# Down-projections of two steps at a time as seven block products (steps 16 to 27 and 40 to 47), and the finished parts of the up weights kept in DRAM for a second use

## What is computed

```python
a = a / (np.sum(a, axis=-1, keepdims=True) + 1e-09)
x = np.matmul(a, v_all)                       # 2 x 8 heads, 768 tokens -> 1536 x 512
...
for e in range(E):                            # E = 4, w1 512 x 1024, w2 1024 x 512
    h = np.maximum(x @ w1[e], 0.0)
    out += p[:, e:e + 1] * (h @ w2[e])
...
h = x @ w_in                                  # 512 x 2048
g = h * (1.0 / (1.0 + np.exp(-1.702 * h)))
return g @ w_out                              # 2048 x 512
```

## Time and profile before

| what | us |
|---|---|
| median of 3 runs | 838.62 (838.14 to 839.32) |
| the profiled execution, its own time | 837.34 |
| its span, first to last instruction | 835.6 |
| PE busy in the span | 814.5 (97%) |
| POOL, DVE, ACT busy | 556.5, 537.9, 399.3 |

### The profile page before, as it was taken

One profiled execution on the slowest core, in us unless ns is written; L12 is line 12 of the kernel. 1 busy time (PEld: TensorE's weight loads), 2 busy tenths in 40 slices (PEclk: granted clock), 3 DMA queues, 4 the chain that ended last, 5 costly groups with the idle time before them and its releaser, 6 DMA issues.

```text
span 835.6 us, 13851 instructions
## 1 busy us (share of the span) xinstructions
PE 814.5 (97%) x5014; PEld 800.9 (96%) x5014; DVE 537.9 (64%) x1194; ACT 399.3 (48%) x859; POOL 556.5 (67%) x414
## 2 busy tenths in 40 slices
PE   5889999999999999999999999999999999999998
PEld 4688999999999999999999999999999999999998
DVE  6888656666655665665665665665665666666665
ACT  3865454444454454433434344444555554554541
POOL 3688655656655799566566588787488787466450
PEclk9989999999999999999999999999999999999999
DMA  9945233142211122122122121121122122321102
GB/s 281 281 126 189 90 117 106 51 153 74 97 52 70 51 84 89 51 76 95 51 82 90 51 88 65 51 93 59 51 74 79 50 82 72 126 86 67 51 1 76
DMA packets 26420, 74.72 MB, mean 89 GB/s; under 512 B 14704, under 2 KB 15856, under 8 KB 20208
## 3 DMA queue, kind: packets, MB, share of 16 engines
q1 hardware_dynamic: 26352, 73.84, 26.9%
HBM read 70.66 MB, written 3.17 MB: 88 GB/s over the span
## 4 chain that ended last, share of the span: by engine, by line
PE 90%; POOL 3%; ACT 3%; issue 2%; DVE 2%; DMA 1%; SPq 0%; DVEq 0%; ACTq 0%; POOLq 0%
PE bank L1155 29%; PE bank L1157 29%; PE bank L1156 29%; ACT prob L676 1%; PE bank L1110 1%; PE bank L1147 1%; PE bank L1121 1%; DMA v_cols<-v_t 1%; POOL wu_lo L536 1%; POOL wd_lo L548 1%; DVE masked L889 0%; POOL xb_other_lo L572 0%; DVE v_sum L877 0%; POOL wd_lo L564 0%; ACT xb_first_hi L737 0%
## 5 line engine op out<-in xcount | busy, mean ns | idle before, releaser
L957 DVE TENSOR_TENSOR xa<-bank,xa 128x384 f32<-128x384 f32 x352 | 195.8, 557 | 219.9 <-PE bank L1157 215.5
L1155 PE MATMUL bank<-h_hi,wd_hi 128*128 128x384 f32 x768 | 257.3, 335 | 0.3 <-DVE xa L955 0.2
L1157 PE MATMUL bank<-h_lo,wd_hi 128*128 128x384 f32 x768 | 256.7, 334 | 0.0
L1156 PE MATMUL bank<-h_hi,wd_lo 128*128 128x384 f32 x768 | 256.6, 334 | 0.0
L548 POOL TENSOR_TENSOR wd_lo<-stage,wd_hi 128x1024 fp32r<-128x1024 f32 x47 | 113.1, 2406 | 165.5 <-ACT wd_hi L719 165.5
L760 ACT ACTIVATE h_hi<-bank 128x384 fp32r<-128x384 f32 x192 | 94.5, 492 | 230.6 <-DVE bank L990 183.3
L1155 PEld LDWEIGHTS bank<-h_hi,wd_hi 128*128 128x128 f32 x768 | 144.2, 188 | 2.4 <-issue 1.5
L1156 PEld LDWEIGHTS bank<-h_hi,wd_lo 128*128 128x128 f32 x768 | 144.2, 188 | 0.0
L1157 PEld LDWEIGHTS bank<-h_lo,wd_hi 128*128 128x128 f32 x768 | 144.2, 188 | 0.0
L536 POOL TENSOR_TENSOR wu_lo<-stage,wu_hi 128x1024 fp32r<-128x1024 f32 x47 | 113.9, 2424 | 0.2 <-ACT wu_hi L707 0.2
L1155 PE MATMUL bank<-xb_other_hi,wu_hi 128*128 128x384 f32 x336 | 112.3, 334 | 0.3 <-ACT snap L744 0.3
(11 more groups left out here) (79 smaller groups left out, 1271.3 us busy)
## 6 DMA issues: line engine op xcount, KB each, us to landing
stage<-weights SPq DMA_DIRECT2D x48, 1024.0 KB, 4.9
k_win<-k_w SPq DMA_DIRECT2D x8, 720.0 KB, 7.7
v_win<-v_w SPq DMA_DIRECT2D x8, 576.0 KB, 8.7
q_bd<-q_t SPq DMA_DIRECT2D x16, 192.0 KB, 8.2
p_bc<-p_rows SPq DMA_DIRECT2D x8, 384.0 KB, 4.8
v_cols<-v_t SPq DMA_DIRECT2D x6, 384.0 KB, 5.9
out<-xa SPq DMA_DIRECT2D x4, 384.0 KB, 7.6
out<-xa SPq DMA_DIRECT2D x8, 192.0 KB, 1.9
```

The costliest lines, as they stand in the source:

```text
L957: nc.vector.tensor_tensor(at, y_bank(g, t), at, ALU.add).then_inc(y_taken, 1)
L1155: nc.tensor.matmul(dst, w_h, a_h, start=first, stop=False, skip_group_check=True)
L1156: nc.tensor.matmul(dst, w_l, a_h, start=False, stop=False, skip_group_check=True)
L1157: return nc.tensor.matmul(dst, w_h, a_l, start=False, stop=last, skip_group_check=True)
```

## The change

In steps 16 to 27 and 40 to 47 two consecutive steps (an even and the odd one after it) make a pair. Their hidden features together are a 512 x 512 factor, so that the down-projection of both can be done as seven block products too, each in two halves of output features d = 0, 1: 14 blocks of six matmuls (`pair_product`) in place of 16 (`down`). In the odd step of a pair PE does P1 and P5 of the pair between its up products, in the even step after it P3, P6, P2, P7 and P4. Around it:

- `gate` writes the tile to SBUF (`h_raw`) and no longer in place in its bank. ACT makes high parts of the raw tiles (`high_tile`, 6 per pair) and DVE the low ones (`low_tile`), POOL makes four sums of hidden blocks (`sum_hidden`, 128 x 768), ACT and DVE split these (`high_sum`, `low_sum`).
- POOL makes four sums of down-weight blocks per pair (`sum_held`, 128 x 512, in `stage`), ACT and POOL split seven held blocks (`high_held`, `low_held`), in place of `high_down` and `low_down`.
- A result block goes from its bank into `xa` 14 times a pair (`take_product`) and not 16.
- The high and low parts of the up weights of steps 1 to 15 and 32 to 39 are written to DRAM (`store_up`, two transfers of 917 KB a step), and read back for steps 17 to 31 and 40 to 47 (`load_up`), so that ACT and POOL make none there (`sum_weights`, `high_raw`, `low_raw`, `high_sums`, `low_sums` fall away). `load_weights` brings only the down half (512 KB) there.
- The blocks `xb_first` and `xb_last`, which hold the input blocks of phases 0 and 2, hold the hidden blocks of the pairs in phases 1 and 3. So those of phase 2 are prepared in three steps (29 to 31) and not six (26 to 31).
- The down weights of steps 29 and 30 are prepared both in step 29, those of 28 in step 28, 31 in 30.

```diff
-AHEAD = (None, 3, 6, 6)
+AHEAD = (None, 3, 3, 6)
...
+PAIRED = ((MOE_STEPS, 28), (FFN0 + PAIRS_2, STEPS))
...
+TAKES = (("P1", 0), ("P1", 1), ("P5", 0), ("P5", 1),
+         ("P3", 0), ("P3", 1), ("P6", 0), ("P6", 1), ("P2", 0), ("P7", 0), ("P7", 1), ("P2", 1), ("P4", 0), ("P4", 1))
+IN_PAIR = 4
...
+ADDED = {"P1": (0, 0, True), "P5": (1, 1, True), "P3": (0, 1, True), "P6": (0, 1, False), "P2": (0, 0, False),
+         "P7": (1, 1, False), "P4": (1, 0, True)}
+
+HELD_2 = ("P1", "P5", "P3", "P6", "P2", "P7", "P4")
+
+TILES_2 = ((0, "C11"), (0, "C21"), (1, "C11"), (1, "C22"), (1, "C21"), (1, "C12"))
...
+        def down_due(g):
+
+            due = [x for x in (g, g + 1) if x < STEPS and not paired(x)]
+            return [x for x in due if (x == g) == (x > 0 and (paired(x - 1) or (x > 1 and paired(x - 2))))]
...
             def load_weights(g):
 
-                wait_count(sp, dnlo_done, g - 1)
-                sp.dma_start(stage[:, g % 2, :], weights[weight_of(g), :, :]).then_inc(stage_in[g % 2], 16)
+                if g > 1:
+                    if paired(g - 2):
+                        sp.wait_ge(slo_done, len(HELD_2) * (pair_of(g - 2) + 1))
+                    else:
+                        sp.wait_ge(dnlo_done, plain(g - 2))
...
+            def load_up(g):
+
+                sp.wait_ge(up_done, ups(g - 2))
+                before = g - (MOE_STEPS if g < FFN0 else PAIRS_2)
+                sp.wait_ge(wu_stored[g % 2], 32 * max(stores(before), stores(g - 2)))
+                sp.dma_start(wu_hi[:, g % 2, :].bitcast(F32), split[weight_of(g), 0, :, :]).then_inc(wu_in[g % 2], 16)
+                sp.dma_start(wu_lo[:, g % 2, :].bitcast(F32), split[weight_of(g), 1, :, :]).then_inc(wu_in[g % 2], 16)
...
+            def sum_held(g):
+
+                n = 4 * pair_of(g)
+                a11, a12, a22, a21 = (held_source(p) for p in ("P1", "P2", "P4", "P5"))
+                for s in range(2):
+                    pool.wait_ge(stage_in[s], 16 * (g // 2 + 1))
+                nc.gpsimd.tensor_tensor(held_source("P7"), a11, a21, ALU.subtract).then_inc(ssum_done, 1)
+                pool.wait_ge(ssum_done, n + 1)
+                nc.gpsimd.tensor_tensor(a21, a21, a22, ALU.add).then_inc(ssum_done, 1)
+                pool.wait_ge(ssum_done, n + 2)
+                nc.gpsimd.tensor_tensor(held_source("P6"), a21, a11, ALU.subtract).then_inc(ssum_done, 1)
+                pool.wait_ge(ssum_done, n + 3)
+                nc.gpsimd.tensor_tensor(held_source("P3"), a12, held_source("P6"), ALU.subtract).then_inc(ssum_done, 1)
+
+            def low_held(g, name):
...
+            def sum_hidden(g, n):
+
+                at = 4 * pair_of(g)
+                if n == 1:
+                    pool.wait_ge(gated_done, ready(g, "C12"))
+                    wait_count(pool, tlo_done, at - 2)
+                    wait_count(pool, tsum_done, at)
+                    a, b = hidden_block(0, 1), hidden_block(0, 0)
+                elif n == 2:
+                    pool.wait_ge(gated_done, ready(g + 1, "C12"))
+                    pool.wait_ge(tlo_done, at + 1)
+                    a, b = hidden_block(1, 1), hidden_sum(1)
+                elif n == 3:
+                    pool.wait_ge(tsum_done, at + 1)
+                    a, b = hidden_block(1, 1), hidden_block(0, 1)
+                else:
+                    pool.wait_ge(tsum_done, at + 2)
+                    pool.wait_ge(blo_done, len(TILES_2) * pair_of(g) + TILES_2.index((1, "C21")) + 1)
+                    a, b = hidden_block(1, 0), hidden_sum(2)
+                nc.gpsimd.tensor_tensor(hidden_sum(n), a, b, ALU.subtract).then_inc(tsum_done, 1)
+
             spread_key_maxima(0)
...
+                if second(g):
+                    sum_hidden(g - 1, 1)
+                    low_held(g - 1, "P3")
+                    low_held(g - 1, "P6")
+                    low_held(g - 1, "P2")
+                    low_held(g - 1, "P7")
+                    low_held(g - 1, "P4")
+                elif paired(g - 1):
+                    sum_hidden(g - 2, 2)
+                    sum_hidden(g - 2, 3)
+                    sum_hidden(g - 2, 4)
...
+                if paired(g) and not second(g):
+                    sum_held(g)
+                    low_held(g, "P1")
+                    low_held(g, "P5")
...
+                for x in down_due(g):
+                    low_down(x)
...
+            def high_tile(g, c):
+
+                g0 = g - g % 2
+                act.wait_ge(gated_done, ready(g, c))
+                if paired(g0 - 1):
+                    act.wait_ge(y_done, taken(g0 - 2, {(0, "1"): "P1", (1, "1"): "P2", (1, "2"): "P3"}[g % 2, c[2]], 1))
+                else:
+                    act.wait_ge(up_done, ups(g0 - 1))
+                nc.scalar.activation(moved_tile(g, c)[0], hidden_raw(g, c), ACT.Copy).then_inc(bhi_done, 1)
...
+            def high_sum(g, n):
+
+                act.wait_ge(tsum_done, 4 * pair_of(g) + n)
+                if paired(g - 1):
+                    act.wait_ge(y_done, taken(g - 2, ("P5", "P6", "P7", "P4")[n - 1], 1))
+                else:
+                    act.wait_ge(up_done, ups(g - 1))
+                nc.scalar.activation(moved_2(n + 1)[0], hidden_sum(n), ACT.Copy).then_inc(thi_done, 1)
...
+            def low_tile(g, c):
+
+                dve.wait_ge(bhi_done, len(TILES_2) * pair_of(g) + TILES_2.index((g % 2, c)) + 1)
+                hi, lo = moved_tile(g, c)
+                nc.vector.tensor_tensor(lo, hidden_raw(g, c), hi.bitcast(F32), ALU.subtract).then_inc(blo_done, 1)
+
+            def low_sum(g, n):
+
+                dve.wait_ge(thi_done, 4 * pair_of(g) + n)
+                hi, lo = moved_2(n + 1)
+                nc.vector.tensor_tensor(lo, hidden_sum(n), hi.bitcast(F32), ALU.subtract).then_inc(tlo_done, 1)
...
+            def pair_product(g, name, d):
+
+                n = len(TILES_2) * pair_of(g)
+                if name in ("P1", "P2", "P3"):
+                    pe.wait_ge(blo_done, n + {"P1": 2, "P2": 5, "P3": 6}[name])
+                else:
+                    pe.wait_ge(tlo_done, 4 * pair_of(g) + {"P5": 1, "P6": 2, "P7": 3, "P4": 4}[name])
+                pe.wait_ge(slo_done, len(HELD_2) * pair_of(g) + HELD_2.index(name) + 1)
+                if name in ("P1", "P5"):
+                    pe.wait_ge(y_taken, taken(g - 2, {"P1": "P4", "P5": "P2"}[name], d) if paired(g - 1) else takes(g))
+                else:
+                    pe.wait_ge(y_taken, taken(g, {"P3": "P5", "P6": "P3", "P2": "P3", "P7": "P6", "P4": "P7"}[name], d))
+                hi, lo = moved_2(MOVED[name])
+                w_hi, w_lo = held_2(name)
+                for f in range(2):
+                    w = slice(BW * f + P * d, BW * f + P * (d + 1))
+                    last = three(pair_bank(name, d), w_hi[:, w], w_lo[:, w], hi[:, f, :], lo[:, f, :],
+                                 name in ("P1", "P5", "P2") and f == 0, f == 1)
                 last.then_inc(y_done, 1)
 
...
+                if second(g):
+                    product(g, "P1")
+                    pair_product(g - 1, "P1", 0)
+                    product(g, "P2")
+                    product(g, "P5")
+                    product(g, "P6")
+                    pair_product(g - 1, "P1", 1)
+                    product(g, "P7")
+                    pair_product(g - 1, "P5", 0)
+                    product(g, "P4")
+                    pair_product(g - 1, "P5", 1)
+                    product(g, "P3")
+                    continue
+                if paired(g - 1):
+                    product(g, "P1")
+                    product(g, "P2")
+                    product(g, "P5")
+                    pair_product(g - 2, "P3", 0)
+                    product(g, "P6")
+                    pair_product(g - 2, "P3", 1)
+                    pair_product(g - 2, "P6", 0)
+                    product(g, "P7")
+                    pair_product(g - 2, "P6", 1)
+                    pair_product(g - 2, "P2", 0)
+                    pair_product(g - 2, "P7", 0)
+                    product(g, "P4")
+                    pair_product(g - 2, "P7", 1)
+                    pair_product(g - 2, "P2", 1)
+                    pair_product(g - 2, "P4", 0)
+                    product(g, "P3")
+                    pair_product(g - 2, "P4", 1)
+                    continue
                 product(g, "P1")
                 down(g - 1, 0)
...
-            for t in range(8):
-                down(STEPS - 1, t)
+            for name, d in TAKES[IN_PAIR:]:
+                pair_product(STEPS - 2, name, d)
```

More of the change, by code:

```diff
@@ L860, in _ @@
                     act.wait_ge(table_in, 1)
+            for n in (2, 3, 4):
+                high_sum(STEPS - 2, n)
         @block.vector
@@ L1078, in _ @@
                 take_y(g - 1, 6)
-                low_hidden(g, "C22")
-                low_hidden(g, "C21")
+                if paired(g):
+                    low_tile(g, "C21")
+                else:
+                    low_hidden(g, "C22")
```

(1 more changed line is left out.)

410 lines of the change are left out of this document (340 added, 70 removed).

## The result

The changed kernel takes **846.36 us** in the median (844.79 to 848.16, four runs), the kernel before 838.53 us on the same chip (838.14 to 839.32): a ratio of 1.0101, 95% interval 1.0082 to 1.0119. The prediction was 847.0, range 834 to 856. The profiled execution took 844.79 us, with a span of 842.9 against 835.6.

The account below looks back on a forecast made before the run. PE's matmul count was taken as the bound: -20.8 us for removed matmuls, +7.5, +7.3, +6.0, +4.4, +1.6 and +3.0 for waits and clock, +9.0 in sum; 846.3 for the profiled execution, 847 forecast for the median, range 834 to 856.

Parts of the forecast that it names:

- The sum: Whole kernel: all gains and losses add to +9.0 us on the profiled 837.3, plus 1.3 for the median over that execution.
- What bounds the kernel: Middle of the kernel: only the number of matmuls on PE sets the time, six matmuls per 1.04 us block.
- Turns between DVE and POOL: DVE operations with two SBUF inputs and POOL instructions each wait for the other's whole instruction; ten meet 15 per pair.
- The steady pair: Even steps 18 to 28: PE waits 1.0 us at P3, 0.1 and 0.2 at P6 and P7; +7.5 us in all.
- being 0.4 late from turns in that step: Odd step of a pair: DVE reaches `add_c12` at 12.0 us, 0.4 late, so `gate` ends at 13.1.
- Steps 42 to 46: Steps 42, 44, 46: a sigmoid delays `gate`; PE waits 2.15 us at P3, 0.3 behind; 2.4 each, +7.3.
- The end, and step 30: After the last up product: P3 5.3 us late, P6 1.1, net +6.0; `down(29, 0)` waits for low down weights, +4.4.
- Steps 31 and 32: Step 31: `sum_weights` of step 32 starts 6.3 us in, ACT's `high_raw` delays `keep`, PE's P7 waits; +1.6 us.
- In step 30 POOL runs on late: Step 30: `low_down` until 23.4 us, then five operations of 1.85, make POOL late for the up weights of step 32.
- The clock: After the two long stops of 4.4 and 5.3 us, PE runs at half clock, 1.5 us lost each; +3.0.
- Transfers: Reloads of up parts: due 12.4 us after being asked for, landing in 9, covered by 3.4 us; cost nothing.
- The rival of late up weights: Nine even steps wait for reloads that exceed 12.4 us; at 14.4 that is +18, 865 us; chance 0.1.

## Why the prediction was right

**The sum.** 847 against 846.4, and in the profiled execution +9.0 against +7.3. The largest single errors are 3.1 us in steps 18 to 28 and 1.8 in steps 42 to 46, both too much, and the end has 0.9 too much; they are met by 3.2 us that it did not have (step 42's transfer, the start, the 0.1 behind each stop, less the stop gone in step 16), by 0.4 more of half clock and by the 0.6 that is missing in the table's sum. The 1.3 us that the prediction added for the median over the profiled execution came out too, as 1.6, and no term of it says why it should. So that the two medians agree within 0.6 us is luck; that the terms add up to within 1.7 us is not, for each long stop is where it was put.

**What bounds the kernel.** Right: PE at its pace. With no sums on POOL the six P3 stops of steps 18 to 28, 4.4 us, are gone and the profile is 4.4 us shorter there; with up products ahead other stops took their place, and the gain is what was left.

**Turns between DVE and POOL.** Right, and shown: with the sums on 8 columns, and with the sum put behind the low part, the low part of C12 takes 0.56 in place of 1.71 to 1.75. In the second POOL still makes its sums in full, only later, so it is not their work but their time that counts. The trace shows the end of DVE's operation 0.4 us behind the end of POOL's, and the rule of the Trainium skill ("SBUF — State Buffer", section "SBUF: two separate sides") that a DVE operation with two SBUF inputs and POOL exclude each other for the whole instruction agrees. It works both ways: POOL is held as well, 2.56 for 1.85.

**The steady pair.** The place was right (P3, all six steps), the size not: 0.70 in place of 1.0 and no wait at P6 and P7. The step that was off is "being 0.4 late from turns in that step": `gate` ends at 383.60, 12.9 into the odd step, not 13.1, and from there on POOL, ACT and DVE run as worked out. P6 and P7 had been given 0.1 and 0.2, which is less than the same error.

**Steps 42 to 46.** 2.15 was expected at P3; 1.17 is measured there, and 1.0 in 44 and 46 at up P5, which waits for the gate behind the sigmoid. I had followed the gate's lateness only to P3, past a product that waits for it sooner: a mis-sized term at P3 and a missing place, whose sum is 2.17. In step 42 it is the late reload that PE waits for in place of the gate.

**The end, and step 30.** 5.4 and 4.2 us against 5.3 and 4.4: both were worked out from the order of instructions and the rows of before, and both vanish with the edit that takes their cause. P6 was given 1.1 more at the end and doesn't wait.

**Steps 31 and 32.** The number was right (1.6 against 1.7), and so was the last part of the chain: POOL comes to `sum_weights` of step 32 at 563.47, 5.97 us into step 31 (6.3 was said), ACT waits for it in `high_raw`, and `keep`, which PE needs, stands behind that:

```profile
563.47 0.74 POOL L700 TENSOR_TENSOR w_sum<-stage 128x256 f32<-128x256 f32 x1
```

```profile
565.05 1.06 ACT L961 ACTIVATE wu_hi<-stage 128x1024 fp32r<-128x1024 f32 x1 [5.42 <-POOL stage L702]
566.02 0.47 ACT L1019 ACTIVATE h_hi<-bank 128x384 fp32r<-128x384 f32 x1
566.38 0.48 ACT L1003 ACTIVATE snap<-bank 128x384 f32<-128x384 f32 x1
```

What fell is why POOL is late, "In step 30 POOL runs on late", behind the late weights of step 29: the 5.97 stands in the kernel without pairs and in that with early down weights as well. In all of them POOL first waits 3.1 us for ACT's high part of a moved block, which stands behind the high parts of that step's tiles and down weights, and so keeps PE's pace; before, with the moved blocks made earlier, `sum_weights` began 1.6 us into the step. With `keep` ahead of `high_raw` the stops are gone.

**The clock.** Two stretches of 1.5 us expected, 1.56 and 1.81 measured, behind the two long stops, and none behind stops of 0.7. (The "ten products of step 0" of the prediction are ten matmuls.) "TensorE: Matmul & The Clock Gate", section "What's actually happening", in the Trainium skill lets the clock fall in an idle engine, and the trace agrees; stops of 1 us left the clock alone in this kernel, but not in each of the others, as the last section shows.

**Transfers.** "Covered by 3.4 us" was wrong once: I counted the time from when a step's products free the buffer, and not what SP has ahead of the reload. By the edit it is SP's order, and with it mended the gate behind it is the wait. The rival of late up weights fell with this: in no kernel here does PE wait for a reload in another step than 42, and there at most 2.6 us.

## What to carry to other kernels

Work taken off a saturated engine is a gain only where its inputs are ready by its own pace: here 14 of the 20.8 us went to three places at the edges of the paired stretches (the step behind, a transfer behind others, the last step), and those are where to leave the trick out. When a stall is covered, look at what is queued behind the waiting instruction on the feeding engine: four times the wait came back at a later product. And where DVE has an operation with two inputs in SBUF while POOL works, add what is left of POOL's instruction to its time; in the one case where the order of the two was changed, another operation was late in its place, at a higher price.
